# A one-core Strassen feed-forward kernel with a Fourier mixing stage: VectorE's two-input subtractions get one input from PSUM

## The reference, cut to what matters

```python
a = softmax(q k^T / 8 + slopes * dist, local window of 96 and 8 global keys)      # batch 2, 8 heads, 768 x 64
x = (a v) put together to [2, 768, 512]
u = x + (x^T @ U @ V)^T                      # first block: mixing over the sequence, rank 32
x = u + relu(u @ w_ch1) @ w_ch2              # 512 -> 2048 -> 512
mixed = real(fft(fft(x, axis=1), axis=2))    # second block: Fourier mixing, over 768 and over 512
u = x + mixed
un = (u - mean(u)) / sqrt(var(u) + 1e-6)     # over the 512 columns
out = u + relu(un @ w2_ch1) @ w2_ch2
```

## Time and profile before

| | us |
|---|---|
| median of 3 runs | 752.55 |
| lowest and highest | 748.69, 754.32 |
| the profiled execution, its own time | 751.75 |
| its span in the profile | 750.0 |
| PE busy in the span | 696.1 |
| DVE, POOL, ACT busy | 438.2, 382.3, 309.8 |

### The profile page before, as it was taken

The page is one execution under the profiler, slowest core; times in us unless marked ns, Lnnn a source line. Parts: engine busy times, 40 slices in busy tenths (PEclk is TensorE's granted clock), DMA queues, the critical chain, the costliest instruction groups (busy, mean ns, idle before and its releaser), DMA issues.

```text
span 750.0 us, 10293 instructions
## 1 busy us (share of the span) xinstructions
PE 696.1 (93%) x3672; PEld 612.6 (82%) x3672; DVE 438.2 (58%) x903; ACT 309.8 (41%) x665; POOL 382.3 (51%) x373
## 2 busy tenths in 40 slices
PE   8989999999999896898897989998997989999998
PEld 6989889989999784787686878877776978899886
DVE  7546564554454767546565578645666476554445
ACT  4667674424343451332342354322432454333421
POOL 0131333345557996334443987445343887665621
PEclk9999999999999999899998999999999999999999
...
GB/s 236 132 123 116 109 89 125 58 57 56 57 67 121 57 92 44 41 30 57 28 57 28 58 57 84 43 42 56 29 57 28 57 57 76 64 79 63 56 113 85
DMA packets 50532, 54.07 MB, mean 72 GB/s; under 512 B 4432, under 2 KB 37328, under 8 KB 50352
## 3 DMA queue, kind: packets, MB, share of 16 engines
...
...
## 4 chain that ended last, share of the span: by engine, by line
PE 63%; DVE 14%; POOL 12%; issue 5%; ACT 4%; DMA 1%; SPq 0%; DVEq 0%; ACTq 0%; POOLq 0%
PE yP L756 8%; PE yP L758 8%; PE yP L757 8%; POOL WCL L517 4%; PE Yb L735 3%; PE Yb L737 3%; PE Yb L736 3%; PE aP L624 3%; PE aP L650 2%; PE Xb L735 2%; PE Zb L735 2%; PE Zb L737 2%; PE Zb L736 2%; PE Xb L736 2%; PE Xb L737 2%
## 5 line engine op out<-in xcount | busy, mean ns | idle before, releaser
L517 POOL TENSOR_TENSOR WCL<-w_stage,WCH 128x512 fp32r<-128x512 f32 (+1 forms) x128 | 154.1, 1229 | 207.0 <-ACT WCH L959 207.0
L1256 DVE TENSOR_TENSOR Y<-yP,Y 128x512 f32<-128x512 f32 x192 | 129.5, 685 | 105.7 <-PE yP L758 105.0
L756 PE MATMUL yP<-WOH,hidH 128*128 128x512 f32 x384 | 159.0, 414 | 22.6 <-DVE Y L1256 22.2
L758 PE MATMUL yP<-WOH,hidL 128*128 128x512 f32 x384 | 156.3, 407 | 0.0
L757 PE MATMUL yP<-WOL,hidH 128*128 128x512 f32 x384 | 155.5, 405 | 0.0
L523 POOL TENSOR_TENSOR WOL<-o_stage,WOH 128x512 fp32r<-128x512 f32 x64 | 85.2, 1353 | 79.7 <-ACT WOH L966 79.7
L756 PEld LDWEIGHTS yP<-WOH,hidH 128*128 128x128 f32 x384 | 74.6, 194 | 43.4 <-DVE Y L1256 22.7
L969 ACT ACTIVATE hidH<-Xb 128x384 fp32r<-128x384 f32 x64 | 31.4, 491 | 188.6 <-PE yP L758 173.8
L758 PEld LDWEIGHTS yP<-WOH,hidL 128*128 128x128 f32 x384 | 74.8, 195 | 17.0
L757 PEld LDWEIGHTS yP<-WOL,hidH 128*128 128x128 f32 x384 | 75.1, 196 | 11.8
L1249 DVE SCALAR_TENSOR_TENSOR hidL<-Xb,hidH 128x384 fp32r<-128x384 f32 x64 | 35.2, 551 | 56.7 <-ACT hidH L969 56.5
...
## 6 DMA issues: line engine op xcount, KB each, us to landing
w_stage<-w_in SPq DMA_DIRECT2D x128, 128.0 KB, 2.4
...
```

Source lines behind the costliest of these rows:

```text
L517: nc.gpsimd.tensor_tensor(WCL[:, g % 2, u0:u1, :, :], w_stage[:, 1 + u0:1 + u1, :, :], hi32(WCH[:, g % 2, u0:u1, :, :]), ALU.subtract).the ...
L756: nc.tensor.matmul(bank[:, :], hh, WOH[:, h % 2, f, :], start=f == 0, stop=False)
L758: mm = nc.tensor.matmul(bank[:, :], hl, WOH[:, h % 2, f, :], start=False, stop=f == 1)
L1256: nc.vector.tensor_tensor(y, yP[t % 2][:, :], y, ALU.add).then_inc(s_yadd, 1)
```

## The change

1. **Split of U.** Before the cast of a factor, ACT copies both of its 128x384 halves into PSUM (banks aP[0], aP[1], aP[2] in turn, `n % 3`). DVE makes the remainder in two subtractions of 384 columns, each with the raw value from PSUM and the high part from SBUF. A copy waits for the subtraction three before it.
2. **Fold.** ACT copies the second half of Y, and its mirror image, into aP[0] and aP[1]; DVE's sums take one input from there, and the results that were MIR and the final EO lie in aP[1] and aP[2]. EX, F0 and the edge's input lie in PSUM too.
3. **Combine.** DIF and SUM lie in aP[1] and aP[2], in place of what the transform left there; PE's next `dim` therefore waits for both combines of the tile row (`s_u2`) in place of DIF and SUM alone.
4. **Second table** in its own buffer CDraw: SP loads it one round earlier with no wait, and the fold doesn't wait for its remainder any more; `mid` and the first `dim` do.
5. **Slots.** fold of m = 1 in three slots of its own, seq 0,1 at slot 7 (round 9), the tile rows at 20 + 8i in place of 18 + 7i, and turn two slots behind its norm in place of one, so at gaps 5 and 6 (behind P2 and L2) of rounds 12, 13 and 14, and of 20, 21 and 22.

The diff, cut to its core:

```diff
+        EDGE = aP[0][:, BLK:BLK + 2 * HT].rearrange("p (t n) -> p t n", t=HT)
+        EX = aP[0][:, BLK + 2 * HT:BLK + 6 * HT].rearrange("p (j t n) -> p j t n", j=2, t=HT)
+        F0 = aP[1][0:1, BLK:BLK + P]
+        DIF, SUM = (aP[i][:, 0:DS + 1] for i in (1, 2))
...
             for n, *what in ((0, "fold", 0, 0), (1, "fold", 0, 1), (2, "fold", 0, 2), (3, "split", 0), (4, "edge"), (6, "seq", 0, 0),
-                             (7, "fold", 1, 0), (8, "seq", 0, 1), (8, "fold", 1, 1), (9, "fold", 1, 2), (10, "split", 1),
-                             (12, "seq", 1, 0), (13, "seq", 1, 1), (15, "seq", 2, 0), (16, "mid")):
+                             (7, "seq", 0, 1), (9, "fold", 1, 0), (10, "fold", 1, 1), (11, "fold", 1, 2), (12, "split", 1),
+                             (14, "seq", 1, 0), (15, "seq", 1, 1), (16, "seq", 2, 0), (18, "mid")):
                 at(n, *what)
-            for n in range(18, 42):
+            for n in range(20, 46):
                 for i in range(HT):
-                    for late, *what in ((0, "dim", i, 0), (1, "dim", i, 1), (2, "combine", i, 0), (3, "stats", i, 0), (4, "combine", i, 1),
-                                        (5, "stats", i, 1), (6, "norm", i, 0), (7, "norm", i, 1), (7, "turn", i, 0), (8, "turn", i, 1)):
-                        if n == 18 + 7 * i + late:
+                    for late, *what in ((8, "turn", i, 0), (9, "turn", i, 1), (0, "dim", i, 0), (1, "dim", i, 1), (2, "combine", i, 0), (3, "stats", i, 0),
+                                        (4, "combine", i, 1), (5, "stats", i, 1), (6, "norm", i, 0), (7, "norm", i, 1)):
+                        if n == 20 + 8 * i + late:
...
-                if g == FPAIRS:
-                    sp.wait_ge(s_csplit, 2 * HT)
-                    sp.dma_start(CSraw[:, 0:DIM_COLS + DC], dim_dft).then_inc(s_cload, 16)
+                if g == FPAIRS - 1:
+                    sp.dma_start(CDraw[:, :], dim_dft).then_inc(s_dload, 16)
...
-                    pe.wait_ge(s_ucl, splits(CHANGES.index(g)) + j + 1)
+                    pe.wait_ge(s_ucl, lo_splits(CHANGES.index(g)) + KF * (j + 1))
...
                     if n == 0:
-                        pe.wait_ge(s_csplit, 2 * HT + KF)
+                        pe.wait_ge(s_csplit, 2 * HT)
+                    if m == 0 and part == 0:
+                        pe.wait_ge(s_exl, b + 1)
...
-                    if i > 0 and part == 0:
-                        pe.wait_ge(s_ds, 2 * (HT * b + i))
+                    if i == 0 and part == 0:
+                        pe.wait_ge(s_csplit, 2 * HT + KF)
+                    elif part == 0:
+                        pe.wait_ge(s_u2, 4 * (HT * b + i))
...
+                for k in range(KF):
+                    n = KF * j + k
+                    if n >= 3:
+                        act.wait_ge(s_ucl, lo_splits(c) + n - 2)
+                    elif n == 0 and c == 0:
+                        act.wait_ge(s_ymix, ymixes(len(MIX)))
+                    elif n == 0:
+                        act.wait_ge(s_u2, 4 * HT * c)
+                    nc.scalar.copy(aP[n % 3][:, 0:BLK], factor(op)[:, k, :])
                 nc.scalar.copy(UCH[:, op, :, :], factor(op)).then_inc(s_uch, 1)
...
+                if what == "fold":
+
+
+                    m, part = at
+                    d, first = slice(P * m, P * m + P), int(m == 0)
+                    if part == 0:
+                        if m == 0:
+                            act.wait_ge(s_yadd, TILES_OUT * FPAIRS * (b + 1))
+                            act.wait_ge(s_csplit, 2 * HT)
+                            act.wait_ge(s_ucl, lo_splits(b + 1))
+                            nc.scalar.copy(EDGE, yb[:, :, D // 2:D // 2 + 2])
+                        else:
+                            act.wait_ge(s_tl, SEQS * b + 2)
+                        nc.scalar.copy(aP[0][:, 0:BLK].rearrange("p (t d) -> p t d", t=HT), yb[:, :, d]).then_inc(s_fy, 1)
+                    elif part == 1:
+                        mirror = slice(D - P * m - first, D - P * m - P, -1)
+                        nc.scalar.copy(aP[1][:, 0:BLK].rearrange("p (t d) -> p t d", t=HT)[:, :, first:P], yb[:, :, mirror]).then_inc(s_fy, 1)
...
-                    nc.scalar.copy(F0H[:, P * m:P * m + P], F0[:, P * m:P * m + P])
-                    nc.scalar.copy(EOH[:, :, :, :], EO[:, :, :, :]).then_inc(s_eoh, 1)
+                    nc.scalar.copy(F0H[:, P * m:P * m + P], F0)
+                    for j in range(2):
+                        mm = nc.scalar.copy(EOH[:, j, :, :], aP[1 + j][:, 0:BLK].rearrange("p (t d) -> p t d", t=HT))
+                    mm.then_inc(s_eoh, 1)
...
-                nc.vector.tensor_tensor(UCL[:, op, :, :], factor(op), hi32(UCH[:, op, :, :]), ALU.subtract).then_inc(s_ucl, 1)
+                for k in range(KF):
+                    n = KF * j + k
+                    nc.vector.tensor_tensor(UCL[:, op, k, :], aP[n % 3][:, 0:BLK], hi32(UCH[:, op, k, :]), ALU.subtract).then_inc(s_ucl, 1)
...
+                    fold = [aP[i][:, 0:BLK].rearrange("p (t d) -> p t d", t=HT) for i in range(3)]
                     if part == 0:
                         if n > 0:
                             dve.wait_ge(s_eol, n)
+                        dve.wait_ge(s_fy, 2 * n + 1)
+                        nc.vector.tensor_tensor(EO[:, 0, :, :], ya[:, :, d], fold[0], ALU.add)
+                        nc.vector.tensor_tensor(EO[:, 1, :, :], ya[:, :, d], fold[0], ALU.subtract).then_inc(s_mir, 1)
                         if m == 0:
-                            dve.wait_ge(s_csplit, 2 * HT + KF)
-                            dve.wait_ge(s_yadd, TILES_OUT * FPAIRS * (b + 1))
-                        nc.vector.tensor_tensor(EO[:, 0, :, :], ya[:, :, d], yb[:, :, d], ALU.add)
-                        nc.vector.tensor_tensor(EO[:, 1, :, :], ya[:, :, d], yb[:, :, d], ALU.subtract)
+                            e = slice(D // 2, D // 2 + 2)
+                            nc.vector.tensor_tensor(EX[:, 0, :, :], ya[:, :, e], EDGE, ALU.add)
+                            nc.vector.tensor_tensor(EX[:, 1, :, :], ya[:, :, e], EDGE, ALU.subtract).then_inc(s_ex, 1)
                     elif part == 1:
+                        dve.wait_ge(s_fy, 2 * n + 2)
                         if first:
-                            nc.vector.memset(MIR[:, :, :, 0:1], 0.0)
-                        nc.vector.tensor_tensor(MIR[:, 0, :, first:P], ya[:, :, mirror], yb[:, :, mirror], ALU.add)
-                        nc.vector.tensor_tensor(MIR[:, 1, :, first:P], ya[:, :, mirror], yb[:, :, mirror], ALU.subtract).then_inc(s_mir, 1)
+                            for i in (1, 2):
+                                nc.vector.memset(fold[i][:, :, 0:1], 0.0)
+                        nc.vector.tensor_tensor(fold[2][:, :, first:P], ya[:, :, mirror], fold[1][:, :, first:P], ALU.subtract).then_inc(s_mir, 1)
+                        dve.wait_ge(s_mir, 4 * n + 2)
+                        nc.vector.tensor_tensor(fold[1][:, :, first:P], ya[:, :, mirror], fold[1][:, :, first:P], ALU.add).then_inc(s_mir, 1)
                     else:
-                        dve.wait_ge(s_mir, 2 * n + 1)
-                        nc.vector.tensor_tensor(F0[:, d], EO[0:1, 1, 0, :], MIR[0:1, 1, 0, :], ALU.add).then_inc(s_mir, 1)
-                        nc.vector.tensor_tensor(EO[:, 0, :, :], EO[:, 0, :, :], MIR[:, 0, :, :], ALU.add)
-                        dve.wait_ge(s_mir, 2 * n + 2)
-                        nc.vector.tensor_tensor(EO[:, 1, :, :], EO[:, 1, :, :], MIR[:, 1, :, :], ALU.subtract).then_inc(s_eo, 1)
+                        dve.wait_ge(s_mir, 4 * n + 3)
+                        nc.vector.tensor_tensor(F0, EO[0:1, 1, 0, :], aP[2][0:1, 0:P], ALU.add).then_inc(s_mir, 1)
+                        nc.vector.tensor_tensor(fold[1], EO[:, 0, :, :], fold[1], ALU.add)
+                        dve.wait_ge(s_mir, 4 * n + 4)
+                        nc.vector.tensor_tensor(fold[2], EO[:, 1, :, :], fold[2], ALU.subtract).then_inc(s_eo, 1)
                 elif what == "split":
                     m, = at
                     n = KF * b + m
                     d = slice(P * m, P * m + P)
                     dve.wait_ge(s_eoh, n + 1)
-                    nc.vector.tensor_tensor(F0L[:, d], F0[:, d], hi32(F0H[:, d]), ALU.subtract)
-                    nc.vector.tensor_tensor(EOL[:, :, :, :], EO[:, :, :, :], hi32(EOH[:, :, :, :]), ALU.subtract).then_inc(s_eol, 1)
+                    nc.vector.tensor_tensor(F0L[:, d], F0, hi32(F0H[:, d]), ALU.subtract)
+                    for j in range(2):
+                        mm = nc.vector.tensor_tensor(EOL[:, j, :, :], aP[1 + j][:, 0:BLK].rearrange("p (t d) -> p t d", t=HT), hi32(EOH[:, j, :, :]), ALU.subtract)
+                    mm.then_inc(s_eol, 1)
...
-                        nc.vector.tensor_tensor(DIF[:, :], aP[1][:, 0:DS + 1], Qs[:, :], ALU.subtract).then_inc(s_ds, 1)
-                        nc.vector.tensor_tensor(SUM[:, :], aP[1][:, 0:DS + 1], Qs[:, :], ALU.add).then_inc(s_ds, 1)
```

(32 more changed lines are left out.)

9 lines of the change are left out of this document (3 added, 6 removed).

## The result

| | before | after |
|---|---|---|
| median us | 753.19 | 710.67 |
| lowest to highest, 4 runs each | 748.69 to 754.32 | 708.26 to 712.65 |
| the profiled execution: its own time, span | 751.75, 750.0 | 711.38, 709.5 |

The ratio is 0.9445, with a 95% interval of 0.9395 to 0.9494: 5.6% faster. 712 was forecast, in a range of 699 to 730.

The account below looks back on a forecast made before the run. PE, 93% busy, bounds the kernel; only its idle time and clock can give. Stage gains 24.4 and 12.4 plus splits 6.5 make 43.3, less 3 for clock, net 40; 751.75 - 40 = 711.5, plus 0.8 for the median: 712, range 699 to 730.

Parts of the forecast that it names:

- the floor: Each Fourier stage with no PE wait and full clock: 115 us, read from the second stage's 135.2.
- second turns, three: Turn at gap 6, behind L2: PE waits for a relu and ACT's copy of the first turn, 1.2 us, three times a stage.
- The split: Stretches before rounds 8, 16 and 24: the new split of U gains 2.2 us each, 6.5 for three.
- the sign "17.5 us": Expected sign of success: the stretch before round 8 takes 17.5 us, where it took 19.9.
- The 1.6 for the low clock behind L4: Stretch before a change of U: after a 2.43 us wait, 3.6 us ran at 1.2 GHz, about 1.6 lost.
- two low stretches, 3: Allowance for PE's clock falling after new waits of 1.1 to 1.8 us: 3 us off the gain, leaving net 40.
- B: Rival: ACT is late, its copies cost 0.84 us, splits gain nothing, fold chains are 1 longer: 722 us; chance 0.17.
- C: Rival: PE's clock falls after each new wait, +16 us, 728 us; chance 0.11.
- D: Rival: PSUM input doesn't free DVE from POOL; only the table and turn slots gain, about 20: 732 us; chance 0.04.
- F: Rival: all new waits are hidden too and PE is near its floor: 697 us; chance 0.05.
- E: Rival: slower or no faster; ACT's copy waits for the subtraction three before, delaying relus, 21 splits; 761 at 2 us each; chance 0.03.
- The 65 ns: DVE instructions with a PSUM source dearer by this each, some 100 instructions, 6.5 us of DVE time; not used in the sum.

## Why the prediction was right

**The floor and the stages.** 115 us a stage plus 7.8 of new waits made 122.8; 121.9 and 121.8 came, so the floor was 0.7 too high and the waits 0.2. The parts:

| | forecast | after, first stage |
|---|---|---|
| round 9, L3 and seq 0,0 | 0.65 + 1.1 | 0.45 + 0.78 |
| round 10, seq 1,0 | 1.7 | 1.57 |
| round 11 | 0 | 0 |
| round 12, first turn | 0.6 | 0.59 |
| second turns, three | 1.2 each | 1.40 each |
| sum (forecast with 0.1 for small ones) | 7.8 | 7.6 |

These are distances between matmul starts less the column unit; the waits view has 1.23 for a second turn. The cause that was read out of ACT's list, a copy behind a relu that waits for L2, is shown by the run with the turn a slot later.

**The split.** 6.5 was forecast, 4.3 measured (36.2, 35.5 and 35.5 became 34.3), and 4.1 by the run that undoes it. The mechanism was right: L4 starts 0.7 earlier as walked (its wait fell from 2.4 to 1.5, with a new 0.2 ahead of L3), and P1 waits 0.4 for hidL. The term was mis-sized in two places. First, the prediction's own steps, L4 0.7 earlier, L4 and L5 at 2.8 in place of 4.45, P1 0.5 later, add up to 1.9 a stretch and not to the 2.2 that it took; the stretches gained 1.6, 1.5 and 1.5, so the sign "17.5 us" was missed (18.3). Second, "DVE's additions up to 1 us later, within what the two yP banks allow" was put at nothing and cost 0.3 in rounds 16 and 24.

The 1.6 for the low clock behind L4 is also no gain by itself. In the run with the split undone the wait before L4 is 2.4 in all three stretches, and the clock fell in the first alone; yet that one takes 19.9 us and the others 19.7 and 19.8. Where the clock stayed at 2.4 GHz, P1 waited for hidL instead:

```profile
PE Xb L738 <- DVE hidL L1278: 1.7, 2, 0.9
```

The changed kernel could keep most of the 1.6 because hidL came earlier too: P1 waits 0.4 for it there, not 0.9.

**The clock.** "I allow two low stretches, 3" was wrong: none came. Waits of 1.5 and less left the clock at 2.4 GHz in every stage; in the undone split 1.2 GHz came back behind one wait of 2.4 (0.91 in the first row of that run) and not behind two others of the same length (1.00).

**The sum.** By stages the change gives 25.3 + 13.5 + 4.3 = 43.1 us, my 43.3 before the clock. The span fell by only 40.5, since in this profile the attention part in front ended 2.6 us later, shown by the last matmul of P1 of round 7 in the timelines of before and after:

```profile
239.76 0.33 PE L737 MATMUL Xb<-UCH,WCL 128*128 128x384 f32 x1
```

```profile
242.36 0.33 PE L740 MATMUL Xb<-UCH,WCL 128*128 128x384 f32 x1
```

So the 3 us that I took off for the clock were made up by something that has nothing to do with the change, and part of the closeness of 712 to 710.7 is luck. The gain by stages, 43.3 against 43.1, is no luck of that kind, but it too has errors that cancel: the splits gave 2.2 less than forecast, the two stages 2.0 more.

**The rivals.** B named ACT, with what seems too small a price: it gave 9.5 us for copies of 0.84, which is 0.7 more per split, where the doubled copies cost 17 for 1.0 more per split. It didn't come about because the copies did take 0.48. C, D and F fell: no low clock, no spread in the 42 remainders, waits where they were walked. E's mechanism exists, as the run with unused copies shows, but at 0.7 us.

**Where the gain comes from** (stage lengths, added in this order): table 6.3, slots 19.5, PSUM inputs of fold 8.9 and combine 4.0, split 4.3. The order matters: the slots are worth 19.5 while the inputs are in SBUF, but with PSUM inputs in place the slots of the tile rows are worth 4.0 only. The two cure much of the same lateness of DVE, and no run has the PSUM inputs with all slots as before, so how much the inputs would give alone stays open.

The 65 ns, an estimate from the figures of the Trainium skill ("VectorE: DVE Perf Modes", section "The TRN2 errata"), by which a PSUM source should be dearer did not show: the first two sums of the fold take 0.554 and 0.547 us at the median with one input in PSUM (lines 1342 and 1343), and 0.548 at the shortest with both in SBUF.
